# The gated stage's values and gates in pairs of groups, their last products on the two halves of the array's rows

## The reference

```python
# 1: a recurrence over positions, per batch and head
y[:, :, t] = einsum('bhd,bhde->bhe', rt, state)
Sa = einsum('bhde,bhe->bhd', state, at)
state = state * wt[:, :, None, :] - einsum('bhd,bhe->bhde', Sa, bt) + einsum('bhd,bhe->bhde', vt, kt)
# 2: the gated stage (x: 4 x 768 x 320, w_in: 320 x 1024, w_spatial: 768 x 768)
h = maximum(x @ w_in, 0); u, v = h[..., :512], h[..., 512:]
v_n = (v - mean(v)) / sqrt(var(v) + 1e-6)            # over the 512 features
v_s = einsum('ts,bsd->btd', w_spatial, v_n) + b_spatial[None, :, None]
x = (u * v_s) @ w_out
# 3: one of 8 experts for each token
e = chosen by argmax(x @ w_gate), or the expert before where sigmoid(x @ w_local) >= 0.5
out = p[e] * (maximum(x @ w1[e], 0) @ w2[e])
```

## Time and profile before

| | |
|---|---|
| three runs | 1016.87 to 1017.91 us, median 1017.14 us |
| the profiled execution | 1017.4 us, span of its instructions 1015.7 us |
| TensorE busy | 974.8 us, 96% of the span |
| weight loads (overlap them) | 773.1 us |
| VectorE, ScalarE, GpSimd busy | 482.5, 262.9, 270.7 us |
| gated stage | from about 386 us to about 694 us |

### The profile page before, as it was taken

One profiled execution on the slowest core, in us unless ns is written; L12 is line 12 of the kernel. 1 busy time (PEld: TensorE's weight loads), 2 busy tenths in 40 slices (PEclk: granted clock), 3 DMA queues, 4 the chain that ended last, 5 costly groups with the idle time before them and its releaser, 6 DMA issues.

```text
span 1015.7 us, 51867 instructions
## 1 busy us (share of the span) xinstructions
PE 974.8 (96%) x23581; PEld 773.1 (76%) x23582; DVE 482.5 (48%) x998; ACT 262.9 (26%) x441; POOL 270.7 (27%) x297
## 2 busy tenths in 40 slices
PE   4789999999999999999999999999999999999996
PEld 3679999999998995555555555558889888888884
DVE  6447887788778853223133133162452332323230
ACT  1134444444444442202202202202111111111110
POOL 4435556655665540000020020020151010110101
PEclk9589999999999999999999999999999999999999
DMA  5225433333333321940110110139131111001000
GB/s 143 63 76 183 143 109 108 100 99 110 111 115 94 102 65 45 313 138 1 39 40 1 39 40 0 50 110 319 41 105 33 34 33 32 22 27 39 21 27 3
DMA packets 56903, 80.58 MB, mean 79 GB/s; under 512 B 22114, under 2 KB 36910, under 8 KB 56848
## 3 DMA queue, kind: packets, MB, share of 16 engines
q1 hardware_dynamic: 32816, 58.08, 18.4%
q10 hardware_dynamic: 21008, 13.06, 5.0%
q0 software_dynamic: 3024, 8.72, 2.4%
HBM read 66.99 MB, written 14.45 MB: 80 GB/s over the span
## 4 chain that ended last, share of the span: by engine, by line
PE 94%; issue 2%; DVE 1%; DMA 1%; ACTq 0%; POOL 0%; ACT 0%; POOLq 0%; DVEq 0%
PE ps_D L1442 13%; PE ps_D L199 12%; PE ps_G L1431 8%; PE ps_E L1431 8%; PE ps_B L209 5%; PE ps_E L928 5%; PE ps_G L180 3%; PE ps_E L180 3%; PE ps_G L188 3%; PE ps_E L188 3%; PE ps_D L1011 3%; PE ps_A L902 3%; PE ps_E L926 3%; PE ps_D L962 3%; PE ps_B L902 2%; PE ps_D L902 2%
## 5 line engine op out<-in xcount | busy, mean ns | idle before, releaser
L1442 PE MATMUL ps_D<-room,hT 128*128 x496 | 138.7, 433 | 0.8 <-issue 0.8
L199 PE MATMUL ps_D<-room 128*128 128x384 f32 x384 | 126.3, 488 | 0.7 <-DVE room L264 0.7
L1442 PEld LDWEIGHTS ps_D<-room,hT 128*128 128x128 f32 x496 | 91.8, 190 | 35.7 <-issue 1.3
L199 PEld LDWEIGHTS ps_D<-room 128*128 128x128 f32 x384 | 72.4, 190 | 50.4 <-DVE room L264 1.3
L1393 POOL DMA_INDIRECT out<-y,token x31 | 30.7, 990 | 279.0 <-DVE y L1549 244.7
L522 POOL DMA_INDIRECT sorted_rows<-rows,slot x24 | 24.1, 1004 | 286.3 <-DVE slot L514 280.2
L866 POOL TENSOR_TENSOR room<-room 32x256 f32<-32x256 f32 x96 | 69.4, 723 | 106.3 <-DVE room L1282 100.9
L1532 DVE COPY w_own<-room 128x1024 f32 x62 | 43.5, 701 | 104.7 <-PE ps_G L1431 58.9
L1431 PEld LDWEIGHTS ps_G<-xTt,w_own 128*128 128x128 f32 x744 | 87.7, 192 | 5.3 <-ACT xTt L1478 0.9
L1431 PE MATMUL ps_G<-xTt,w_own 128*128 128x128 f32 x744 | 88.3, 275 | 0.6 <-ACT xTt L1478 0.6
L1431 PE MATMUL ps_E<-xTt,w_own 128*128 128x128 f32 x744 | 88.1, 275 | 0.0
(11 more groups left out here) (211 smaller groups left out, 1526.5 us busy)
## 6 DMA issues: line engine op xcount, KB each, us to landing
room<-in_moe_w SPq DMA_DIRECT2D x8, 1280.0 KB, 12.9
room<-in_moe_w SPq DMA_DIRECT2D x8, 1024.0 KB, 9.5
room<-in_kb SPq DMA_DIRECT2D x48, 160.0 KB
room<-in_vt SPq DMA_DIRECT2D x24, 320.0 KB, 3.0
x_in<-sorted_rows ACTq DMA_DIRECT2D x27, 161.0 KB, 2.2
room<-in_w SPq DMA_DIRECT2D x48, 82.7 KB
room<-in_a SPq DMA_DIRECT2D x48, 80.0 KB
room<-in_r SPq DMA_DIRECT2D x48, 80.0 KB
```

Source lines behind the costliest of these rows:

```text
L199: mm = pe.matmul(self.vs_bank[n % 2][:, 0:TH], self.v[:, s, d * P:(d + 1) * P], self.wspT[:, s, t * TH:(t + 1) * TH], start=(s == 0), stop ...
L1442: mm = pe.matmul(self.ps_y, side.hT[:, u % 2, f, :], self.weights.w2[:, bass.ds(e, 1), f, :], start=(f == 0), stop=(f == self.NF - 1))
```

## The change

Groups of values and gates are issued in pairs. A pair first runs the two whole chunks of its first group, then of its second, each into its own bank, and then the last products of both: 64 rows each, the first on partitions 0 to 63, the second on 64 to 127. For that the last 64 features of x and w_in are loaded a second time, into the rows that were zeros; pad_rows is gone. Pairs use G and E, the two banks of B or the two of D. A pair waits until the relus of the last pair on its banks are done, each relu waits for both groups of its pair, and mix waits at its first product for all relus of its batch. In batch 0 the order is values 0-1, the turn, the scores, values 2-3, the outputs, gates 0-1, 2-3, values 4-5, gates 4-5, 6-7.

```diff
@@ -45,6 +45,7 @@
 TH = SEQ // 2
 ND = D_HALF // P
 GROUPS2 = TILES + 2 * ND
+REST = KCH[-1][1]
 
 
 class Carver:
@@ -92,9 +93,10 @@
         self.stats, self.mv = sb("stats", TILES, 6), sb("mv", TILES, 2)
         self.sd, self.rs, self.half_sd, self.var = (sb(n, TILES) for n in ("sd", "rs", "half_sd", "var"))
         A, B, D, G, E = banks
-        self.h_bank = (G, E.rearrange("p a i t -> p (a i t)"))
+        self.pair_banks = {"GE": (G[:, :], E.rearrange("p a i t -> p (a i t)")), "B": (B[:, 0], B[:, 1]),
+                           "D": (D[:, 0], D[:, 1])}
         self.vs_bank, self.o_bank = (D[:, 0], D[:, 1]), (B[:, 0], B[:, 1])
-        self.transfers = 1 + NK
+        self.transfers = 2 + NK
         self.loaded, self.out_loaded, self.biased = sem("gated_loaded"), sem("out_loaded"), sem("biased")
         self.x_tile, self.x_full = [sem(f"x_tile{i}") for i in range(TILES)], sem("x_full")
         self.h_made, self.h_out = sem("h_made"), sem("h_out")
@@ -106,6 +108,7 @@
         w_in, w_spatial, b_spatial, w_out, w_gate, w_local = self.sources
         pairs = [(self.wspT[:, :, :], w_spatial.rearrange("(t p) s -> p t s", p=P))]
         pairs += [(self.win[0:n, k, :], w_in[lo:lo + n, :]) for k, (lo, n) in enumerate(KCH)]
+        pairs += [(self.win[REST:, NK - 1, :], w_in[DM - REST:, :])]
         dst, src = pairs[part]
         eng.dma_start(dst, src).then_inc(self.loaded, 16)
 
@@ -125,22 +128,18 @@
         for dst, src in pairs:
             eng.dma_start(dst, src).then_inc(self.out_loaded, 16)
 
-    def pad_rows(self, eng, done):
-
-        n = KCH[-1][1]
-        eng.memset(self.xT[n:, NK - 1, :], 0.0).then_inc(done, 1)
-        eng.memset(self.win[n:, NK - 1, :], 0.0).then_inc(done, 1)
-
     def load_tile(self, eng, i):
 
         cols = slice(i * P, (i + 1) * P)
         for k, (lo, n) in enumerate(KCH):
             eng.dma_start(self.xT[0:n, k, cols], self.x_rows[0, lo:lo + n, cols]).then_inc(self.x_tile[i], 16)
+        eng.dma_start(self.xT[REST:, NK - 1, cols], self.x_rows[0, DM - REST:, cols]).then_inc(self.x_tile[i], 16)
 
     def load_x(self, eng, b):
         eng.wait_ge(self.h_made, GROUPS2 * b)
         for k, (lo, n) in enumerate(KCH):
             eng.dma_start(self.xT[0:n, k, :], self.x_rows[b, lo:lo + n, :]).then_inc(self.x_full, 16)
+        eng.dma_start(self.xT[REST:, NK - 1, :], self.x_rows[b, DM - REST:, :]).then_inc(self.x_full, 16)
 
     def fold(self, pe, woutT, wgl, bank, done):
 
@@ -155,44 +154,67 @@
         act.wait_ge(folded, 1)
         act.activation(self.wout[:, :, DM:ROW], bank[:, :, 0:EXPERTS + 1], ACT.Copy).then_inc(done, 1)
 
-    @staticmethod
-    def v_at(b, i):
-
-        return b * GROUPS2 + (i + ND if b == 0 and i == TILES - 1 else i)
-
-    @staticmethod
-    def u_at(b, j):
-
-        return b * GROUPS2 + (TILES - 1 if b == 0 and j < ND else TILES) + j
-
-    def h_group(self, pe, n):
-        if n >= 2:
-            pe.wait_ge(self.h_out, n - 1)
-        return self.h_bank[n % 2]
+    V_FIRST = {0: (0, 1, 4), 1: (0, 1, 2)}
+    U_FIRST = {0: (2, 3, 5, 6), 1: (3, 4, 5, 6)}
+    BANKS = {0: ("GE", "GE", "D", "B", "GE", "D", "B"), 1: ("GE", "B", "GE", "GE", "B", "GE", "B")}
+
+    def v_at(self, b, i):
+
+        return b * GROUPS2 + 2 * self.V_FIRST[min(b, 1)][i // 2] + i % 2
+
+    def u_at(self, b, j):
+
+        return b * GROUPS2 + 2 * self.U_FIRST[min(b, 1)][j // 2] + j % 2
+
+    def banks_of(self, n):
+        return self.BANKS[min(n // GROUPS2, 1)][n % GROUPS2 // 2]
+
+    def bank_of(self, n):
+        return self.pair_banks[self.banks_of(n)][n % 2]
+
+    def until_free(self, pe, n):
+
+        same = [m for m in range(0, n, 2) if self.banks_of(m) == self.banks_of(n)]
+        if same:
+            pe.wait_ge(self.h_out, same[-1] + 2)
+
+    def pair(self, pe, n, width, left, right):
+
+        self.until_free(pe, n)
+        for g in range(2):
+            for k in range(NK - 1):
+                pe.matmul(self.bank_of(n + g)[:, 0:width], left(g, k, slice(0, P)), right(g, k, slice(0, P)),
+                          start=(k == 0), stop=False, skip_group_check=True)
+        for g in range(2):
+            rows = slice(g * REST, (g + 1) * REST)
+            pe.matmul(self.bank_of(n + g)[:, 0:width], left(g, NK - 1, rows), right(g, NK - 1, rows),
+                      start=False, stop=True, skip_group_check=True).then_inc(self.h_made, 1)
 
     def values(self, pe, b, i):
-        if b == 0:
-            pe.wait_ge(self.x_tile[i], 16 * NK)
-        elif i == 0:
-            pe.wait_ge(self.x_full, 16 * NK * b)
-        bank = self.h_group(pe, self.v_at(b, i))
-        for k in range(NK):
-            mm = pe.matmul(bank[:, :], self.xT[:, k, i * P:(i + 1) * P], self.win[:, k, D_HALF:],
-                           start=(k == 0), stop=(k == NK - 1))
-        mm.then_inc(self.h_made, 1)
+
+        for t in (i, i + 1):
+            if b == 0:
+                pe.wait_ge(self.x_tile[t], 16 * (NK + 1))
+        if b >= 1 and i == 0:
+            pe.wait_ge(self.x_full, 16 * (NK + 1) * b)
+        self.pair(pe, self.v_at(b, i), D_HALF,
+                  lambda g, k, rows: self.xT[rows, k, (i + g) * P:(i + g + 1) * P],
+                  lambda g, k, rows: self.win[rows, k, D_HALF:])
 
     def gates(self, pe, b, j):
+
         d, t = j % ND, j // ND
-        bank = self.h_group(pe, self.u_at(b, j))
-        for k in range(NK):
-            mm = pe.matmul(bank[:, 0:TH], self.win[:, k, d * P:(d + 1) * P], self.xT[:, k, t * TH:(t + 1) * TH],
-                           start=(k == 0), stop=(k == NK - 1))
-        mm.then_inc(self.h_made, 1)
+        if b >= 1 and self.banks_of(self.u_at(b, j)) == "B":
+            pe.wait_ge(self.o_out, TILES * b)
+        self.pair(pe, self.u_at(b, j), TH,
+                  lambda g, k, rows: self.win[rows, k, (d + g) * P:(d + g + 1) * P],
+                  lambda g, k, rows: self.xT[rows, k, t * TH:(t + 1) * TH])
 
     def mix(self, pe, b, j):
         d, t, n = j % ND, j // ND, 2 * ND * b + j
         if j == 0:
             pe.wait_ge(self.normed, TILES * (b + 1))
+            pe.wait_ge(self.h_out, GROUPS2 * (b + 1))
         if n >= 2:
             pe.wait_ge(self.vs_out, n - 1)
         for s in range(TILES):
@@ -203,6 +225,8 @@
     def outs(self, pe, b, i):
         n = TILES * b + i
         pe.wait_ge(self.gated, 2 * ND * b + ND * (1 + i * P // TH))
+        if i == 0:
+            pe.wait_ge(self.h_out, GROUPS2 * (b + 1) + (4 if b + 1 < BATCH else 0))
         if n >= 2:
             pe.wait_ge(self.o_out, n - 1)
         for d in range(ND):
@@ -212,13 +236,13 @@
 
     def relu_v(self, act, b, i):
         n = self.v_at(b, i)
-        act.wait_ge(self.h_made, n + 1)
-        act.activation(self.v[:, i, :], self.h_bank[n % 2][:, :], ACT.Relu).then_inc(self.h_out, 1)
+        act.wait_ge(self.h_made, n // 2 * 2 + 2)
+        act.activation(self.v[:, i, :], self.bank_of(n)[:, :], ACT.Relu).then_inc(self.h_out, 1)
 
     def relu_u(self, act, b, j):
         d, t, n = j % ND, j // ND, self.u_at(b, j)
-        act.wait_ge(self.h_made, n + 1)
-        act.activation(self.g[:, d, t * TH:(t + 1) * TH], self.h_bank[n % 2][:, 0:TH], ACT.Relu).then_inc(self.h_out, 1)
+        act.wait_ge(self.h_made, n // 2 * 2 + 2)
+        act.activation(self.g[:, d, t * TH:(t + 1) * TH], self.bank_of(n)[:, 0:TH], ACT.Relu).then_inc(self.h_out, 1)
 
     def roots(self, act, b):
         act.wait_ge(self.stat, (2 * TILES + 1) * (b + 1))
@@ -630,7 +654,7 @@
         eng.wait_ge(self.blank_tile, 16)
 
 
-ZEROED = 15
+ZEROED = 13
 CONSTANTS = 29
 CH = 32
 CHUNKS = SEQ // CH
@@ -1062,29 +1086,26 @@
                 gated.values(pe, 0, 0)
                 pe.wait_ge(vu_done, t.now2)
                 turn_vu(t)
-                gated.values(pe, 0, 1)
                 scores_r(t)
                 gated.values(pe, 0, 2)
                 pe.wait_ge(kt_d, t.now)
                 outputs(t)
-                gated.values(pe, 0, 3)
+                gated.gates(pe, 0, 0)
+                pe.wait_ge(y_d, CHUNKS + 1)
+                gated.gates(pe, 0, 2)
                 gated.values(pe, 0, 4)
-                for j in range(ND):
-                    gated.gates(pe, 0, j)
-                gated.values(pe, 0, 5)
-                for j in range(ND, 2 * ND):
-                    gated.gates(pe, 0, j)
+                gated.gates(pe, 0, ND)
+                gated.gates(pe, 0, ND + 2)
                 for j in range(2 * ND):
                     gated.mix(pe, 0, j)
-                pe.wait_ge(y_d, CHUNKS + 1)
                 for b in range(1, BATCH):
-                    for i in range(TILES):
+                    for i in range(0, TILES, 2):
                         gated.values(pe, b, i)
                     for i in range(TILES):
                         gated.outs(pe, b - 1, i)
-                    for j in range(2 * ND):
+                    for j in range(0, 2 * ND, 2):
                         gated.gates(pe, b, j)
-                        if j == 5:
```

(7 more changed lines are left out.)

## The result

| | before | after |
|---|---|---|
| median | 1017.0 us (4 runs, 1016.18 to 1017.91) | 1023.41 us (4 runs, 1022.34 to 1024.3) |
| ratio | | 1.0062, 95% interval 1.0045 to 1.008 |
| profiled execution, its span | 1017.4, 1015.7 us | 1023.11, 1021.4 us |
| gated stage in the profile, first values to first expert product | 308.0 us | 314.6 us |

The change made the kernel 6.4 us slower, where 1.5 us was forecast. The time is above the range given. The page of the changed kernel, against the earlier trace rows: the matrix work has a smaller share of the chain, "issue" a larger one, and the clock has one slice of 8 in the middle, where there was none.

A forecast was written before the change was run, and what follows sets the result against it. TensorE's stream was taken as the bound. Streaming -20.6, switches about +10.2, three holes +8.8, batch 0's hole +1.2, copy +1.1 and late tile +0.8 gave +1.5 us: 1018.6 us, range 1013.4 to 1022.5.

The forecast's parts named there:

- the clock falls in the holes: Rival: TensorE's clock halves around the idle holes before mixing, 1.7 us a fall; 1020.3 us for one, 1022.0 for two; chance 0.15.
- The holes' own length: Before mixing in batches 1 to 3, TensorE streams nothing for 2.92 us while waiting for relu 7; +8.8 us for three.
- Batch 2: Like batches 1 and 3: columns, switches and hole take 31.36 us against 31.0, a loss of 0.36 us.
- The overlap: Last products of a pair run side by side on row halves, saving two parts a pair; -20.6 us over four batches.
- strictly in program order: Rival: parts of a pair's last products run in program order, saving one part instead of two; 1028.9 us; chance 0.10.
- The switches: Each change between whole array and row halves costs 0.20 us of drain and open weight load; about +10.2 us.
- The rival of cheap switches: Only the drain shows at a change of array shape, 0.10 us as in the fold; 1013.4 us; chance 0.16.
- Batch 0: First batch of the gated stage: exposed copy, late tile and a hole; mixing starts 0.4 us later than before.
- the late tile: In batch 0, values 4-5 wait 0.8 us for tile 5 of x, its fourth load issued behind three at 0.44 us.
- The hole before its mixing: In batch 0, mixing waits for the last two relus, leaving TensorE a hole of 1.2 us.

The follow-up runs named there:

- hole_filled: The changed kernel with three 128x512 products into an unread bank before mixing's wait in batches 1 to 3; 1019.72 us, ratio 1.0028.
- before_hole: The kernel before, unpaired, but in batches 1 to 3 relu 6 waits for gates 7 and mixing for all relus; 1027.34 us, ratio 1.0106.
- same_half: The changed kernel without mixing's wait for every relu, and with both last products of a pair on rows 0 to 63; 1029.53 us, ratio 1.0127.
- whole_last: The changed kernel without mixing's wait for every relu, and with last products on all 128 rows, half of them zeros; 1018.17 us, ratio 1.0012.

## Why the prediction was wrong

- **The step that failed** is the rival "the clock falls in the holes". It was left out of the sum, with a chance of 0.15 and 1.7 us a fall. The trace of the changed kernel has two falls around three holes, of 3.04 and 1.69 us, and hole_filled, which keeps the wait and takes away only the idleness, gives 5.0 us of the stage back. The forecast was missed by 4.8 us. The price "half of 3.4 us" was right for the third hole and half of the truth for the first, where the low clock lasted 6.8 us. So even the rival's own 1022.0 for two falls, and with it the range, stayed below the 1023.41 measured. The argument for the small chance leaned on the earlier trace rows, where 1.41 us of TensorE in 3.4 "didn't lower it at once". One row without a fall can't bear that, and in that trace TensorE's last product ended at 1006.5 and the clock did fall at 1011.9. Of the six idle holes of 2.7 to 2.8 us whose clock was read (three each in the changed kernel and in before_hole) three came with the low level; of the three filled ones none did.
- **The holes' own length** was right: 2.74 us in the chain, and 2.92 forecast with a tail and a weight load that the chain counts elsewhere. Batch 2, the only one undisturbed, lost 0.31 us, forecast 0.36.
- **The overlap** was right: starts 0.01 us apart, 1.06 us to the next pair, 20.2 us by same_half against 20.6. The rule of the Trainium skill that was weighed against it ("TensorE: Matmul & The Clock Gate", Part 3) is that matmuls start and end strictly in program order. The prediction applied it to the two parts of an fp32 product; so read, it would have put the next pair 1.5 us after, and 10.3 us into the time. The trace doesn't bear out this reading: the second product's first part starts 0.52 us before the first's second part. Product by product the trace agrees with the rule: G starts at 454.60 and E at 454.61, and their last records end at 455.72 and 455.73. In which order the four parts stand in the program no trace shows.
- **The switches** were right at 0.20 us, by the 0.69 to 0.70 us parts and the 2.64 us for 14 switches between a batch of whole_last and one of same_half. The rival of cheap switches falls. Its row, the fold of the earlier trace rows, was read at half clock; no clock record of that trace reaches back to it, so that reading isn't shown.
- **Batch 0** was right in its places and 0.43 us short in size, mostly the late tile (1.09 us instead of 0.8): the fourth load was issued 0.50 us after the third, not 0.44, and landed 2.1 us after its issue, where 1.9 was taken. The hole before its mixing was 1.09 us, forecast 1.2.
- Without its waits the prediction's own sum stands: 1018.6 less the three holes (8.8) and batch 0's (1.2), and 0.8 for the four switches that then stand in their place, is 1009.4, measured 1009.33. The kernel before stood 0.5 us lower beside that run than in the prediction's base, so the sum is met to within that.

What stays open is why, of holes that look alike, some are followed by the low clock and some not, and why the first fall lasted twice as long as the others. The two falls of the changed kernel began at 495.0 in the hole and at 652.0, 0.4 us after the work had begun again; that of before_hole began 1.2 us after. How often each falls over many executions is known only roughly, from the mean granted clock over each run's whole span. Two falls of together 10.2 us lower it by 5.1/1021 = 0.005. The four runs of the changed kernel have 0.977 to 0.983; ten of hole_filled's twelve have 0.986 or more, 17 of the 22 of the kernel before run beside it 0.985 or more. That fits falls in most executions of the changed kernel, but no more than fits: the profiled execution of before has 0.983 too, and no low clock in its gated stage. Its low clock lies ahead of 70 us and lasts 30.7 us, where that of the changed kernel's trace lasts 20.5 us there and 10.2 us around the holes. The mean can't tell the one from the other.

## What to carry to other kernels

A wait that makes TensorE stand still for a few microseconds costs its length and, with a chance that one can't leave out of the sum, about as much again at half clock (here up to 3.04 us for a hole of 2.74); name it as a term. Before a stage's first product wait only for what its own bank and operands need, and drain what it does need before any table load on ScalarE. Products on half of the rows pay if two run side by side, and pay more if the half-row products of neighbouring groups stand together, because every change of shape cost 0.2 us here.

## What was not expected of the hardware

- The low clock after idle holes of 2.7 us: 6.8 us of it in one case, 3.4 us in two, none in three, and none after holes of 1.0 us or of 2.8 us filled with work.
- Two fp32 products on the two row halves run part against part: starts at 454.60 and 454.61, then 455.13 and 455.14, with hardly any loss: 20.2 us of 20.6 over the stage, 5.11 of 5.16 in a batch.
